# Attention and two expert layers on one core: w1's and w2's split blocks stored from ScalarE's DMA queue in the first third

## The reference

```python
a = x @ w_a; b = x @ w_b            # 512 x 1536
x = a * b @ w_out                   # 1536 x 512
p = domain_probs / (domain_probs.sum(-1, keepdims=True) + 1e-09)
for e in range(4):
    h = np.maximum(x @ w1[e], 0.0)  # 512 x 1024
    out += p[:, e:e + 1] * (h @ w2[e])
```

## Time and profile before

| What | us |
|---|---|
| Median of 3 runs | 1167.03 (1166.7 to 1167.75) |
| The profiled execution | 1166.37 |
| Its span, first to last instruction | 1164.6 |
| PE (TensorE) busy | 1158.1 (99%) |
| DVE (VectorE) busy | 858.1 (74%) |
| ACT (ScalarE) busy | 502.0 (43%) |
| SP's DMA queue, q1: share of 16 engines | 73.8% |

### The profile page before, as it was taken

The page is one execution under the profiler, slowest core; times in us unless marked ns, Lnnn a source line. Parts: engine busy times, 40 slices in busy tenths (PEclk is TensorE's granted clock), DMA queues, the critical chain, the costliest instruction groups (busy, mean ns, idle before and its releaser), DMA issues.

```text
span 1164.6 us, 18783 instructions
## 1 busy us (share of the span) xinstructions
PE 1158.1 (99%) x7595; PEld 1127.5 (97%) x7595; DVE 858.1 (74%) x1154; ACT 502.0 (43%) x877; POOL 0.7 (0%) x6
## 2 busy tenths in 40 slices
PE   9999999999999999999999999999999999999999
PEld 8999998989999889999999999999999999999999
DVE  7786789788787893367877777797346787777778
ACT  6554464445544542244544434344233533333334
POOL 0000000000000000000000000000000000000000
PEclk9999999999999999999999999999999999999999
DMA  7396794879888699939777777748894877776762
GB/s 273 145 347 244 287 353 179 344 278 372 326 313 305 258 414 356 337 122 336 303 270 266 281 285 257 249 166 285 255 362 169 326 262 268 254 266 252 266 253 89
DMA packets 73595, 319.54 MB, mean 274 GB/s; under 512 B 7389, under 2 KB 14501, under 8 KB 57125
## 3 DMA queue, kind: packets, MB, share of 16 engines
q1 hardware_dynamic: 72932, 317.17, 73.8%
q10 hardware_dynamic: 576, 1.18, 0.3%
HBM read 221.81 MB, written 96.51 MB: 273 GB/s over the span
## 4 chain that ended last, share of the span: by engine, by line
PE 94%; DMA 2%; DVE 2%; ACT 1%; issue 1%; SPq 0%; ACTq 0%; DVEq 0%
PE ps L695 21%; PE ps L697 21%; PE ps L696 21%; PE ps L1113 20%; PE ps L1037 10%; DMA kept_w<-w 1%; PE ps L704 1%; PE ps L723 1%; DMA kept_w<-lone 1%; PE ps L712 1%; PE ps L750 0%; PE ps L779 0%; ACT three L1242 0%; SPq L592 0%; PE ps L815 0%
## 5 line engine op out<-in xcount | busy, mean ns | idle before, releaser
L1113 PE MATMUL ps<-hw,w2s 128*128 128x384 f32 x1320 | 231.4, 334 | 0.0
L1113 PEld LDWEIGHTS ps<-hw,w2s 128*128 128x128 f32 x1320 | 229.0, 188 | 0.0
L1242 ACT ACTIVATE ps<-ps 128x384 f32<-128x384 f32 (+1 forms) x185 | 92.1, 503 | 188.5 <-PE ps L697 184.8
L695 PE MATMUL ps<-x,wab 128*128 128x384 f32 x500 | 167.6, 335 | 0.3 <-ACT ps L1242 0.3
L697 PE MATMUL ps<-x,wab 128*128 128x384 f32 x500 | 167.1, 334 | 0.0
L696 PE MATMUL ps<-x,wab 128*128 128x384 f32 x500 | 167.0, 334 | 0.0
L1242 ACT ACTIVATE hw<-xraw 128x768 fp32r<-128x768 f32 x112 | 94.6, 846 | 135.3 <-DVE xraw L2366 58.5
L695 PE MATMUL ps<-x,w1s 128*128 128x384 f32 x448 | 151.1, 337 | 0.0
L697 PE MATMUL ps<-x,w1s 128*128 128x384 f32 x448 | 149.7, 334 | 0.0
L696 PE MATMUL ps<-x,w1s 128*128 128x384 f32 x448 | 149.7, 334 | 0.0
L1037 PE MATMUL ps<-w,h 128*128 128x512 f32 x576 | 133.0, 391 | 0.5 <-ACT h L1537 0.5
(11 more groups left out here) (215 smaller groups left out, 1844.9 us busy)
## 6 DMA issues: line engine op xcount, KB each, us to landing
wab<-kept_ab SPq DMA_DIRECT2D x70, 512.0 KB, 5.4
w1s<-kept_w SPq DMA_DIRECT2D x32, 1024.0 KB, 6.4
w2s<-kept_w SPq DMA_DIRECT2D x16, 2048.0 KB, 7.5
w1s<-kept_w SPq DMA_DIRECT2D x16, 1536.0 KB, 6.2
w2s<-kept_w SPq DMA_DIRECT2D x16, 1536.0 KB, 6.2
kept_ab<-wab SPq DMA_DIRECT2D x42, 512.0 KB, 6.2
raw<-in_w SPq DMA_DIRECT2D x16, 1024.0 KB, 10.2
kept_w<-w SPq DMA_DIRECT2D x16, 1024.0 KB, 12.8
```

What stands on the lines that cost most here:

```text
L695: pe.matmul(dst, stat(HI), mov(HI), start=first, stop=False, skip_group_check=True)
L1113: return pe.matmul(ps[:, first_bank + s, 0:N], w2s[:, n, w_part, at:at + P], hw[:, H_PLACE[n], h_part, kt, :], start=begins, stop=ends, sk ...
L1242: return act.activation(dst, src, ACT.Copy)
```

## The change

The stores of w1's and w2's split blocks are taken out of SP's list and put into ScalarE's. w1's three stand at the beginning of a window's list on ScalarE, behind a wait for w1_lo; w2's three stand behind the high parts of h's C11, behind a wait for w2_lo. Loads, and the stores of `three` and `lone`, stay with SP. SP keeps both waits, w1_lo and w2_lo. Two waits are new, in the second third's first pair, ahead of what overwrites the tiles: ScalarE waits for w2_kept before a_sb, VectorE for w1_kept and w2_kept before `pair_g`.

```diff
@@ first_windows (SP)
                     if w < PH - 1:
                         load_w1(w + 1)
                     else:
                         load_ab(0)
-                    for n in range(3):
-                        sp.dma_start(kept_w1[w, :, w1_part(n)], w1[:, w1_part(n)].bitcast(F32)).then_inc(w1_kept, 16)
                     sp.wait_ge(w2_lo, 2 * w + 2)
-                    for b, at in ((0, 1), (1, 5), (3, 6)):
-                        sp.dma_start(kept_w2[w, :, at], w2[:, :, b, :].bitcast(F32)).then_inc(w2_kept, 16)
@@ run_pair (ScalarE)
                 next_ab(4)
+                if T == 1 and j == 0:
+                    act.wait_ge(w2_kept, 48 * PH)
@@ ScalarE
+            def store_w1(w):
+                act.wait_ge(w1_lo, 3 * w + 3)
+                for n in range(3):
+                    act.dma_start(kept_w1[w, :, w1_part(n)], w1[:, w1_part(n)].bitcast(F32)).then_inc(w1_kept, 16)
+
+            def store_w2(w):
+                act.wait_ge(w2_lo, 2 * w + 2)
+                for b, at in ((0, 1), (1, 5), (3, 6)):
+                    act.dma_start(kept_w2[w, :, at], w2[:, :, b, :].bitcast(F32)).then_inc(w2_kept, 16)
+
             def first_phase(w):
 
                 Q = set_e(0, w)
                 t = TILES + w
+                store_w1(w)
                 if w in (1, 3, 5):
                     exp(t - 1)
                     exp(t)
...
                 for s in range(2):
                     act.wait_ge(p2_made, 2 * Q + s + 1)
                     hi_h("C11", s, ps[:, BA[s], 0:N])
+                store_w2(w)
                 if w == PH - 1:
                     round_sum(1, XA12)
@@ run_pair (VectorE)
+                if T == 1 and j == 0:
+                    dve.wait_ge(w1_kept, 48 * PH)
+                    dve.wait_ge(w2_kept, 48 * PH)
                 pair_g(T, j, "C11")
```

## The result

The changed kernel takes 1184.99 us (median of 5 runs, 1184.41 to 1186.92), the kernel before 1166.98 us (5 runs). The ratio is 1.0159, 95% interval [1.0148, 1.017]: slower by 18 us. The forecast was 1180.0 us with a range of 1170.5 to 1187.0.

A forecast was written before the change was run, and what follows sets the result against it. The prediction took TensorE as the bound, busy 1158.1 of 1164.6 us. Losses of 10.0, 0.5 and 2.4 us, 12.9 together, on 1166.37 gave 1179.3, and 0.66 for the median 1180.0; range 1170.5 to 1187.

The forecast's parts named there:

- Nothing to win: In the windows TensorE waits once, 0.48 us in w = 7; earlier splits win nothing beyond part of that.
- The head start: In w = 6, w1's stores on ScalarE overtake the stores of three and lone by 3.7 us.
- The landing of lone: In w = 6, lone lands at 369.6 in place of 364.2, sharing bandwidth with w1; w2's sum on VectorE starts 4.6 us late.
- TensorE's waits in even windows: Late lone delays w2's sums and h; TensorE loses 3.8, 2.8, 3.4 us in w = 2, 4, 6, sum 10.0.
- Odd windows: In w = 1, 3, 5 w2's sums come after h, so the loss is 0, with up to 1 us.
- ScalarE's issues: Three issues take 1.75 us on ScalarE: loss 0.5 us in w = 0, 2.4 in w = 7, elsewhere hidden.
- the wait for the seed that I expected: In w = 7, w1's issues delay the first seed to 395.2, where TensorE needs it at 394.39.
- The sum: Over the windows, 10.0 us from late sums plus 0.5 in w = 0 and 2.4 in w = 7: 12.9 us.
- the third rival: After waits of 3 to 4 us TensorE's clock falls, adding 2.8 us three times: 1188 us; chance 0.08.
- the low end: Three issues on ScalarE take 0.9 us if they run beside the ACTIVATE dispatched before them.

The follow-up runs named there:

- the dose: The changed kernel with one more 1024 KB store behind w1's in w = 2, 4, 6: 1193.96 us, ratio 1.0232.
- the one-queue run: The kernel before, all stores on SP, but w1's for w = 1 to 6 issued ahead of three and lone: 1180.40 us, ratio 1.0117.
- only w2's with the consumer moved: The changed kernel with w1's stores back on SP and VectorE making w2's sums behind h in even windows too: 1181.24 us, ratio 1.0128.
- only w1's: The changed kernel with w2's stores back on SP at their old place, w1's staying on ScalarE: 1182.86 us, ratio 1.0137.

## Why the prediction was right, and where it was not

- **Nothing to win**: right. TensorE waited nowhere that the change relieves; ScalarE's waits for w1's stores vanished without effect.
- **The head start**: said 3.7 us, measured 3.7 in w = 6.
- **The landing of lone**: said 369.6 - 357.17 = 12.4 us after its issue in w = 6, measured 12.8; the dose and the one-queue run show that the bytes ahead of it make it, and the rate was 368 GB/s where 371 were taken.
- **TensorE's waits in even windows**: said 3.8, 2.8 and 3.4 us, measured 5.01, 2.45 and 3.08; 10.0 in sum, measured 10.5. w = 2 was sized too small by 1.2 us. I let w1_lo come 0.5 us sooner there, and it came at the same time (224.82): w1's load, landing 17.0 us after its issue in place of 10.2, had held up w = 1's sums by 1.39 us. The rest is lone, which took 13.2 us to land.
- **Odd windows**: said 0, right.
- **ScalarE's issues**: in w = 7 said 2.4, measured 1.8 (a wait of 2.27 us in place of 0.48), near it partly by luck, since two errors cancel. I took 1.75 us for each three issues. w1's took 1.82 and held ScalarE up by only 0.44, and the wait for the seed that I expected didn't come; w2's took 3.11, not 1.75. With only w2's stores on ScalarE they took 2.50 there, so w1's ahead of them on the queue explain a part at most. In w = 0 said 0.5, measured 0.3, but not at p6, where w1's issues cost nothing: the wait stands before the second part, behind w2's. In w = 1 to 6 they hid in slack as said.
- **The sum**: 12.9 us forecast, 12.2 of more idle time measured. That step held.
- **The clock**: the third rival, given 0.08, came true together with the forecast, and should have been a term of it. The forecast's sum had set the price of a wait at the wait itself. Measured, 6.4 us of slower matmuls on top; I gave 8.4 as its price, 2.8 for each even window, where w = 2, 6 and 7 paid 2.1, 3.2 and 1.6 and w = 4 nothing. The waits of 5.01, 3.08 and 2.27 us were followed by matmuls at the lower clock, the one of 2.45 us was not. By the Trainium skill, TensorE: Matmul & The Clock Gate (table in "Why this matters for your kernels"), idle gaps between bursts of matmuls are to be avoided, since they take the clock back to its lower level; the first three agree. Of the 18 us the forecast named 13; the other 5 are this. They fell inside the range only because its upper end, 1187, left room for larger waits.

## What to carry to other kernels

A store is not free because nobody computes on it: ask which transfer it is put ahead of, who waits for that one, and what slack that consumer has. The order of transfers in a nearly full DMA system is a schedule, and a second queue gives part of it away. When TensorE's slack is used up, look at whether a wait brings down its clock, and price the matmuls behind it too.

## What the runs showed of the hardware that I had not expected

DMA issues on ScalarE can run beside the ACTIVATE before them. In the changed kernel's w = 7 w1's three start with the ACTIVATE that stands ahead of them, and the next ACTIVATE comes only 0.44 us after that one's end; w2's three, which stand behind a wait for VectorE, find none to hide beside and cost in full:
```profile
406.08 1.49 ACT L1238 ACTIVATE three<-three_f 128x1536 fp32r<-128x1536 f32 x1 [8.83 <-DVE lone_f L2216]
406.09 1.82 ACTq L1554 DMA_DIRECT2D kept_w<-w  x3
408.01 0.97 ACT L1238 ACTIVATE ps<-ps 128x384 f32<-128x384 f32 x2 [0.44 <-issue]
...
416.16 3.11 ACTq L1559 DMA_DIRECT2D kept_w<-w  x3
419.32 0.85 ACT L1238 ACTIVATE x<-xf_later 128x768 fp32r<-128x768 f32 x1 [3.69 <-issue]
```
I had named this as the low end only, since no row of before showed it.

A wait's length alone didn't tell whether the clock falls after it. Waits of 2.27 us (changed kernel, w = 7) and 2.82 us (the one-queue run, w = 6) were followed by the lower clock; waits of 2.45 us (changed kernel, w = 4) and 2.94 us (only w2's with the consumer moved, w = 7, and only w1's, w = 6) were not. The same changed kernel was granted 0.993 to 0.998 on the mean in its five runs, with times from 1184.41 to 1186.92.
